# Pair blocks with one output column range: the second product's two weight parts summed on TensorE, the row and the turned weights on ScalarE

## The reference

```python
# 1. softmax over 7 taps per head, causal sliding sum over the sequence
out = einsum('hk,bskhg->bshg', softmax(weight), x_windows)
# 2. soft mixture: 32 slots, dispatch by softmax over tokens, combine by softmax over slots
slot_input = d.T @ x;  h = relu(slot_input[e] @ w1[e]);  slot_out[e] = h @ w2[e];  x = c @ slot_out
# 3. top-2 mixture: 8 experts, F = 1024, noisy gate
for e in range(8):
    for k in range(2):
        h = relu(x[mask] @ w1[e]);  out[mask] += top2_w[mask, k] * (h @ w2[e])
```

## Time and profile before

| what | value |
|---|---|
| median of 3 runs | 989.81 us (989.12 to 990.42) |
| the profiled execution | 991.08 us |
| its span, first to last instruction | 989.2 us |
| mean granted TensorE clock | 0.957 |
| PE, DVE, ACT, POOL busy | 925.8, 622.0, 462.4, 342.2 us |

### The profile page before, as it was taken

The page is one execution under the profiler, slowest core; times in us unless marked ns, Lnnn a source line. Parts: engine busy times, 40 slices in busy tenths (PEclk is TensorE's granted clock), DMA queues, the critical chain, the costliest instruction groups (busy, mean ns, idle before and its releaser), DMA issues.

```text
span 989.2 us, 26078 instructions
## 1 busy us (share of the span) xinstructions
PE 925.8 (94%) x7942; PEld 731.9 (74%) x7943; DVE 622.0 (63%) x1381; ACT 462.4 (47%) x975; POOL 342.2 (35%) x362
## 2 busy tenths in 40 slices
PE   5999989995798889999999999999999999999995
PEld 5999989991464337778777777777777777777774
DVE  5222352446456877888777767776777777677773
ACT  2222221221124445555566556666655665565663
POOL 5000000001001003333445555554556565656652
PEclk9999989997769798999999999999999999999998
DMA  7457776787634103333333333333334444444441
GB/s 235 129 159 210 219 233 200 267 276 194 182 83 118 49 25 82 88 96 93 106 107 112 107 111 109 110 110 104 109 113 111 104 114 107 109 110 112 109 112 33
DMA packets 75148, 127.51 MB, mean 129 GB/s; under 512 B 10540, under 2 KB 43772, under 8 KB 73176
## 3 DMA queue, kind: packets, MB, share of 16 engines
q1 hardware_dynamic: 58936, 108.78, 36.9%
q0 software_dynamic: 15248, 17.49, 8.9%
q10 hardware_dynamic: 912, 0.52, 0.2%
HBM read 63.49 MB, written 16.86 MB: 81 GB/s over the span
## 4 chain that ended last, share of the span: by engine, by line
PE 90%; DVE 3%; DMA 2%; issue 1%; ACT 1%; another core or an unknown queue 0%; POOL 0%; ACTq 0%; PEldq 0%; SPq 0%; DVEq 0%
PE ps L1449 30%; PE ps L1453 15%; PE ps L1428 11%; PE ps L1181 10%; PE ps L1230 4%; PE ps L1232 4%; PE ps L1345 3%; PE ps L1403 3%; PE ps L1174 3%; PE ps L1418 2%; PE ps L1324 1%; DMA gate_room<-in_moe_w 1%; PE ps L1265 1%; DMA a_room<-in_moe_w 1%; PE ps L1482 1%
## 5 line engine op out<-in xcount | busy, mean ns | idle before, releaser
L655 ACT ACTIVATE x_ring<-ps 128x512 f16<-128x512 f32 x472 | 256.8, 599 | 212.0 <-PE ps L1428 174.4
L1449 PE MATMUL ps<-w2hl,x_ring 128*128 x1888 | 347.2, 327 | 2.6 <-DVE x_ring L1124 0.9
L1114 DVE SCALAR_TENSOR_TENSOR x_ring<-ps,x_ring 128x512 f16<-128x512 f32 x472 | 303.1, 684 | 10.8 <-ACT x_ring L655 3.2
L1449 PEld LDWEIGHTS ps<-w2hl,x_ring 128*128 128x128 f16 x1888 | 176.4, 97 | 98.6 <-issue 9.2
L522 POOL DMA_INDIRECT stage<-pay_rows,row_id x151 | 150.7, 998 | 282.7 <-PE ps L1428 162.1
L1453 PE MATMUL ps<-w2hl,x_ring 128*128 x1888 | 195.0, 246 | 1.1 <-DVE x_ring L1114 1.1
L532 POOL DMA_INDIRECT out_rows<-x_ring,row_id x151 | 170.1, 1127 | 58.5 <-issue 44.2
L1453 PEld LDWEIGHTS ps<-w2hl,x_ring 128*128 128x128 f16 x1888 | 163.3, 98 | 32.2 <-DVE x_ring L1114 1.9
L1428 PE MATMUL ps<-c,x_ring 96*128 96x128 f16 x1888 | 145.4, 220 | 0.5 <-DVE c L1107 0.5
L1107 DVE COPY c<-ps 96x256 f16<-96x256 f16 (+1 forms) x151 | 38.9, 257 | 146.1 <-PE ps L1418 128.7
L1428 PEld LDWEIGHTS ps<-c,x_ring 96*128 96x128 f16 x1888 | 122.5, 98 | 1.2 <-issue 0.9
(11 more groups left out here) (303 smaller groups left out, 683.2 us busy)
## 6 DMA issues: line engine op xcount, KB each, us to landing
x_ring<-a_room SPq DMA_DIRECT2D x236, 192.0 KB
x_ring<-in_x SPq DMA_DIRECT2D x14, 1536.0 KB, 6.6
stage<-in_moe_w SPq DMA_DIRECT2D x26, 768.0 KB, 9.3
a_room<-in_moe_w SPq DMA_DIRECT2D x12, 768.0 KB, 11.3
gate_room<-in_moe_w SPq DMA_DIRECT2D x8, 768.0 KB, 10.7
stage<-pay_rows,row_id POOLq DMA_INDIRECT x151
out_rows<-x_ring,row_id POOLq DMA_INDIRECT x151
pay_rows<-x_ring SPq DMA_DIRECT2D x1, 1904.0 KB, 5.9
```

The lines of the kernel that those rows point to most:

```text
L655: a.activation(hh[:, m % 2, 4 * half:4 * half + 4, :].rearrange("p j q -> p (j q)"), ps[:, 2 + 2 * (m % 2) + half, :], ACT.Relu).then_inc( ...
L1114: last = v.scalar_tensor_tensor(hl[:, m % 2, 4 * half:4 * half + 4, :].rearrange("p j q -> p (j q)"), ps[:, 2 + 2 * (m % 2) + half, :], 0. ...
L1449: t_.matmul(ps[:, 6 + b % 2, 0:2 * D], hh[:, m % 2, j, :], w, start=k == 0 and j == 0, stop=False)
```

## The change

`LIGHT = PRE - 1` is 18. In blocks 0 to 17:

- the second product streams w2-high and w2-low as two matmuls of 192 columns into the same PSUM columns 0 to 191, with hh's slice j as weights for each;
- ScalarE scales those 192 columns straight into the row (`whole_row`), and neither `y_lo` nor VectorE's `row_sum` is used. `ylo_ready` is therefore counted from block 18 on;
- ScalarE copies the turned combine weights of blocks 2 to 17 (`turned`), behind relu(m+1) and ahead of `split_high`; VectorE keeps the copies of blocks 0, 1 and 18 on.

```diff
--- before.py
+++ after.py
@@ -60,6 +60,7 @@
     LC = NB - FP
     LB = (N - FP * P + (E - 1) * (P - 1)) // P
     PRE = FP - 2 * LB
+    LIGHT = PRE - 1
     NBK = FP + 2 * LB
     NPASS = 2 * NBK - 2 * LB
     LG = -(-LC // 8)
@@ -655,6 +656,20 @@
                     a.activation(hh[:, m % 2, 4 * half:4 * half + 4, :].rearrange("p j q -> p (j q)"),
                                  ps[:, 2 + 2 * (m % 2) + half, :], ACT.Relu).then_inc(hh_ready, 1)
 
+            def whole_row(b):
+
+                act.wait_ge(o_ps, pass_of(b + 1))
+                if b >= 4:
+                    act.wait_ge(y_out[b % 4], b // 4 * 16)
+                a.activation(y[:, b % 4, :], ps[:, 6 + b % 2, 0:D], ACT.Copy, scale=sc(SC_UN)).then_inc(y_ready, 1)
+
+            def turned(b):
+
+                act.wait_ge(c3_ps, b + 1)
+                act.wait_ge(h_ps, pass_of(b - 1))
+                a.activation(c3[:, b % 2, :, :].rearrange("p k q -> p (k q)"), ps[0:KS, 0, 0:P].bitcast(F16), ACT.Copy
+                             ).then_inc(c3_ready, 1)
+
             def low_sum(i, b):
                 act.wait_ge(o_ps, i * 12 + pass_of(b + 1))
                 wait(act, y_ready, i * 8 + (b - 1))
@@ -677,10 +692,14 @@
 
             def blk(i, b):
                 m = pass_of(b)
-                if b:
+                if b > LIGHT:
                     low_sum(i, b - 1)
+                elif b:
+                    whole_row(b - 1)
                 if m + 1 < NPASS:
                     relu(i, m + 1)
+                if b + 2 < LIGHT:
+                    turned(b + 2)
                 if b + LEAD < NBK:
                     split_high(i, b + LEAD)
                 if is_pair(b):
@@ -1118,7 +1137,7 @@
                 last.then_inc(hl_ready, 1)
 
             def row_sum(i, b):
-                dve.wait_ge(ylo_ready, i * 8 + (b + 1))
+                dve.wait_ge(ylo_ready, i * 8 + (b + 1 - LIGHT))
                 if b >= 4:
                     dve.wait_ge(y_out[b % 4], turns(i, b - 4, 4) * 16)
                 v.scalar_tensor_tensor(y[:, b % 4, :], ps[:, 6 + b % 2, 0:D], sc(SC_UN), y_lo[:, b % 2, :],
@@ -1144,11 +1163,11 @@
                 m = pass_of(b)
                 if b + 2 < NBK and not is_pair(b):
                     c_out(i, b + 2)
-                if b:
+                if b > LIGHT:
                     row_sum(i, b - 1)
                 if m + 1 < NPASS:
                     low(i, m + 1)
-                if b + 2 < NBK and is_pair(b):
+                if LIGHT <= b + 2 < NBK and is_pair(b):
                     c_out(i, b + 2)
                 if b + LEAD < NBK:
                     split_low(i, b + LEAD)
@@ -1445,8 +1464,14 @@
                 for half in range(2):
                     pe.wait_ge(hh_ready, i * 24 + (2 * m + half + 1))
                     for j in range(4 * half, 4 * half + 4):
-                        w = w2hl[:, bass.ds(e, 1), j, :].rearrange("p a d -> p (a d)")
-                        t_.matmul(ps[:, 6 + b % 2, 0:2 * D], hh[:, m % 2, j, :], w, start=k == 0 and j == 0, stop=False)
+                        if b < LIGHT:
+                            for lo in range(2):
+                                w = w2hl[:, bass.ds(e, 1), j, lo * D:(lo + 1) * D].rearrange("p a d -> p (a d)")
+                                t_.matmul(ps[:, 6 + b % 2, 0:D], hh[:, m % 2, j, :], w,
+                                          start=k == 0 and j == 0 and lo == 0, stop=False)
+                        else:
+                            w = w2hl[:, bass.ds(e, 1), j, :].rearrange("p a d -> p (a d)")
+                            t_.matmul(ps[:, 6 + b % 2, 0:2 * D], hh[:, m % 2, j, :], w, start=k == 0 and j == 0, stop=False)
                 pe.wait_ge(hl_ready, i * 12 + (m + 1))
                 for j in range(FJ):
                     w = w2hl[:, bass.ds(e, 1), j, 0:D].rearrange("p a d -> p (a d)")
```

## The result

The changed kernel takes 997.42 us (median of 4 runs, 997.29 to 998.35) beside 989.96 us for the kernel before in the same comparison: ratio 1.0078, 95% interval 1.0061 to 1.0096, so 7.5 us slower by the medians (7.7 by the ratio). The forecast was 991.2 in a range up to 996.0. The time lies above that range. What was forecast was 1.4 us, within what the measurement calls no change; what came is a clear loss, and of the size that rival 1 gave, "4 to 8 us".

The account below looks back on a forecast made before the run. The prediction took the columns PE streams to bound the changed stage. Column split +0.7, sequencer +1.1 and both engine moves -0.4 gave +1.4 us on the timed median of 989.81: forecast 991.2 us, range 989.0 to 996.0.

Parts of the forecast that it names:

- rival 1: Light blocks' computed addresses: PE's sequencer becomes the bound, 4 to 8 us slower, about 995; chance 0.30.
- Bound by PE's columns: Stage from 372 to 480 us: paced by the columns PE streams; DVE work counts only through two waits, 1.1 us.
- Column split: High halves of 18 blocks: 288 matmuls of 384 columns become two of 192 each, +0.7 us, bounds 0 and 9.
- PE's sequencer: High halves: 16 address computations a pass instead of 8, 0.13 us apart, use up its lead; +1.1 us, upper bound 4.2.
- So the 14 lookup blocks just hold: Sequencer's lead suffices in the 14 lookup blocks; 0.4 us is missing only after blocks 0 and 10, 0.8 us.
- Row on ScalarE: Row sum leaves DVE, shortening two PE stalls by 0.33 us each; with the copy's delay, about -0.4 us together.
- Copy on ScalarE: Sixteen turned-weight copies leave DVE, worth 0; on ACT nothing waits, but 0.1 us comes off each stall's gain.
- Rival 2: Light blocks: addresses are reused or hidden and the DVE stalls vanish, -0.8 us, 989.0; chance 0.12.
- rival 4: High halves: the second weight load of each pair is not hidden, 9 us bound, 999; chance 0.03.
- rival 5: Low half needs addresses of its own again, 8 more a pass, 37 us, 1028; chance 0.02.
- Rival 3: Light blocks: the copy makes ScalarE's ReLU late for PE, 6.6 us, 996.4; chance 0.07.

Follow-up runs that it names:

- h4: The kernel before with the expert number loaded twice a pass in the first 18 blocks: ratio 0.9994, -0.6 us against before.
- g1: The changed kernel with expert 0 as a constant in the light blocks, so neither expert loads nor address computations: ratio 0.9993, -0.7 us against before.
- a1: The changed kernel with both matmuls of a pair streaming the same 192 columns of w2, so no added addresses: ratio 1.0008, +0.8 us against before.
- e1: The changed kernel with the copies of the turned weights back on VectorE: ratio 1.0019, +1.9 us against before.
- b2: The kernel before with only the column split; row still made in two steps, copies still on VectorE: ratio 1.0048, +4.7 us against before.
- d1: The kernel before with only the copies of the turned weights of blocks 2 to 17 moved to ScalarE: ratio 1.0007, +0.7 us.
- j1: The changed kernel with split_high ahead of the turned-weight copy on ScalarE in the first blocks: ratio 1.0075, +7.3 us against before.
- i1: The changed kernel with one load of both expert numbers per block in the first 18 blocks: ratio 1.0053, +5.2 us against before.

## Why the prediction was wrong, point by point

**Bound by PE's columns.** Right for the kernel before (h4: 36 more loads cost nothing), and no longer so after the change.

**Column split, +0.7.** Right: undisturbed high halves take 1.32 us from start to start (33 of g1's 36), and g1 with all 576 matmuls is level with before. The second weight load is hidden. The line in the Trainium skill ("TensorE: Matmul & The Clock Gate", Back-to-back issue gap) that would give 18 us does not hold for this stream.

**PE's sequencer, +1.1: this term is what failed.** The mechanism was named and the counts were right: 288 more addresses at L1470, none at L1478, 0.132 us apart on average as taken. The step that failed is "So the 14 lookup blocks just hold". It rests on the sequencer's time between the passes: 0.7 us from a first pass's last address to the second pass's first (0.2 + 0.3 + 0.2), and 0.8 from there to the next block's. That made a chain of 30 x 0.13 + 0.7 + 0.8 = 5.4 us a block, just under the array's 5.5. By the starts in the changed kernel's queue the two take 0.84 and 1.16 us on average. The 0.84 is 0.16 to the load, 0.52 to the event and 0.16 to the address. The 1.16 is 0.28, 0.44 and 0.43, with 0.2 of waiting for the ReLU half in it. A block's chain is then 30 x 0.132 + 0.84 + 1.16 = 5.96 us, against the array's 5.50 in a lookup block and 5.00 in one without.

Two lookup blocks (3 and 11) took 6.1 to 6.2 us before the change too, and block 0 took 6.8, so that they had room. For the other 12 and block 10 the estimate is 12 x 0.46 + 0.96 = 6.5 us, where I had 1.1. Measured is the difference between the changed kernel and a1: 5.4 us of stretch, 7.0 by the ratios. I had seen a load of 646 ns in rows 7 and booked 0.3 us in all for such. But the mean over the 36 passes was 0.36 us in the kernel before already, and it is 0.41 and 0.47 in the changed kernel's two profiles. Of a resource that comes out so near the bound, the average of all its parts was needed, not its quickest case. My upper end for the term, 4.2, moved only the spacing and left the loads at their shortest; rival 1, at "expert loads of 0.45", was near them, and deserved more than 0.30.

**Row on ScalarE, -0.4.** About right where the sequencer is no bound: PE's waits for the low part (L1114, now L1133) fell from 1.1 to 0.4 us, and g1's stretch is 0.2 us under before with 0.7 more for the columns, which leaves -0.9. These are single profiles. In the company of the split it gave 2.8 us (e1 beside b2), with expert loads shorter by as much, which no term had.

**Copy on ScalarE, 0.** Right by itself (d1: +0.7, interval with zero). Wrong in the company of the split, where 4 to 6 us hang on it. I had costed each edit against the slack of the kernel before, and the first edit uses that slack up.

**Rivals.** Rival 1 happened. Rival 2 is refuted by the 576 address rows, rival 4 by a1, rival 5 by L1478, which has none of its own. Rival 3 in the form given (PE waits for ScalarE in each block) did not happen; j1 shows that starting the ReLU earlier buys nothing.

**Open.** Why an expert load lasts 0.30 us in one place and 0.73 in another. Over the light stretches of the eleven traced kernels with such loads (all but i1 and g1), the 116 loads with no VectorE hl instruction starting within 0.7 us of them lasted 0.33 us on average. The 93 with one started 0.3 to 0.7 us before them and the next from 0.1 before to 0.3 after their start lasted 0.50, and the other 257 lasted 0.38. That is a correlation for these windows alone. Whether the two share a resource, and which, was not tried.

## What to carry to other kernels

A matmul whose operand address comes from a register costs time on PE's queue that the busy share does not show; count different addresses per pass, add the register loads at their mean length, and compare the sum with the array's time before you cut such matmuls in two. Where two resources come out as close as here (5.4 us a block against 5.5), price each edit again after the first one has used the slack. To find whether a chain is the bound, double a link of it in both kernels: here that gave 11 us in the one and nothing in the other.

## What the runs showed of the hardware that I had not expected

- An address computation is 46 ns long, but the next one comes 0.124 us later in the median and 0.132 on average (540 spacings of the changed kernel), and where the array waits for it, so does the matmul. Pairs that need no new address pass the queue far faster: the eight of a first product lie between two events that are 0.126 us apart at the shortest, in the kernel before and in the changed one.
- The register load of one number lasts 0.30 to 0.73 us in the changed kernel, that of two numbers 0.89 in the median (i1), longer than two single ones at their shortest.
- PE's array can be reported 99% busy (106.84 of 108 us) while its blocks of 6 us are 0.4 us longer on average (7.2 us over 18 blocks), nearly all of it for want of addresses.
